# Last 64 keys of two heads in one transposition and in V's 64x64 quadrants, V's banks moved, all engine lists reordered

## What is computed

```python
# q, k, v: (4, 8, 576, 64) float32; x: (2304, 512); w_in: (512, 2048); w_out: (2048, 512)
q_rot, k_rot = (rotate(q), rotate(k))            # rotary embedding
scores = scale * np.matmul(q_rot, k_rot.transpose(0, 1, 3, 2))
scores = scores - np.max(scores, axis=-1, keepdims=True)
attn = np.exp(scores)
attn = attn / (np.sum(attn, axis=-1, keepdims=True) + 1e-09)
x = np.matmul(attn, v)                           # then to (2304, 512)
h = x @ w_in
sp = np.where(h > 20.0, h, np.log1p(np.exp(np.minimum(h, 20.0))))
g = h * np.tanh(sp)
return (g @ w_out).astype(np.float32)
```

## Time and profile before

| | us |
|---|---|
| median of 3 runs | 639.99 (636.27 to 640.86) |
| the profiled execution | 638.16 |
| its span, first to last instruction | 635.3 |
| attention, to the MLP's first matmul | 238.05 |

### The profile page before, as it was taken

How to read it: one execution, slowest core, us unless ns; L and a number is a source line. 1 busy time by engine, 2 the same in 40 slices (tenths; PEclk the granted TensorE clock), 3 DMA queues, 4 the chain that set the end, 5 groups by cost and what they waited for, 6 DMA issues and landing times.

```text
span 635.3 us, 12674 instructions
## 1 busy us (share of the span) xinstructions
PE 613.1 (97%) x4548; PEld 472.6 (74%) x4548; DVE 337.3 (53%) x573; ACT 430.0 (68%) x693; POOL 260.4 (41%) x208
## 2 busy tenths in 40 slices
PE   3899999999999979999999999999999999999997
PEld 1566666666666659978888888888888888888886
DVE  3777777687788655773433534433434335144331
ACT  2778778787778746757857558665488574586663
POOL 4877688676797368994000620001420006000000
PEclk9999999999999999999999999999999999999999
DMA  5676676576676445130000060000420000000001
GB/s 193 196 227 203 213 214 195 175 211 209 214 214 203 112 130 144 47 87 33 1 0 1 0 166 35 0 1 0 120 78 0 0 0 0 33 33 0 0 0 66
DMA packets 39343, 59.61 MB, mean 94 GB/s; under 512 B 4880, under 2 KB 25104, under 8 KB 39312
## 3 DMA queue, kind: packets, MB, share of 16 engines
q1 hardware_dynamic: 39312, 59.20, 31.2%
HBM read 42.60 MB, written 9.51 MB: 82 GB/s over the span
## 4 chain that ended last, share of the span: by engine, by line
PE 68%; POOL 17%; issue 7%; DMA 3%; SPq 2%; ACT 1%; DVE 1%; POOLq 0%; DVEq 0%; ACTq 0%
PE ps_y L754 10%; PE ps_y L756 10%; PE ps_y L755 10%; PE ps_h L732 9%; PE ps_h L730 9%; PE ps_h L731 9%; POOL raw L492 8%; PE ps_s L622 5%; PE ps_s L679 5%; POOL qk_a L500 2%; PE ps_t L649 2%; POOL win_lo L515 2%; DMA xb_l<-r_early 1%; POOL wout_lo L562 1%; POOL xb_l L556 1%
## 5 line engine op out<-in xcount | busy, mean ns | idle before, releaser
L1032 DVE TENSOR_TENSOR h_sb<-h_sb,m_sb 128x1024 f32<-128x1024 f32 x36 | 55.5, 1542 | 145.5 <-ACT m_sb L893 145.5
L960 DVE TENSOR_SCALAR_CACHE_REDUCE minus_s<-ps_s 128x576 f32<-128x576 f32 x144 | 106.1, 753 | 38.7 <-PE ps_s L622 37.5
L820 ACT ACTIVATE prob<-minus_s,neg_max 128x576 f32<-128x576 f32 x128 | 97.9, 768 | 29.1 <-DVE minus_s L960 29.0
L622 PE MATMUL ps_s<-qk_b,qk_a 64*128 64x288 f32 (+1 forms) x320 | 101.0, 445 | 12.7 <-DMA qk_b<-qk_a 11.0
L754 PE MATMUL ps_y<-wout_hi,gh 128*128 128x512 f32 x288 | 112.2, 389 | 0.5 <-POOL wout_lo L562 0.5
L756 PE MATMUL ps_y<-wout_hi,gl 128*128 128x512 f32 x288 | 112.1, 389 | 0.0
L755 PE MATMUL ps_y<-wout_lo,gh 128*128 128x512 f32 x288 | 112.0, 389 | 0.0
L492 POOL TENSOR_TENSOR raw<-raw,rope_t 128x576 f32<-128x576 f32 x62 | 86.8, 1421 | 49.5 <-DMA raw<-qk_in 49.5
L622 PE MATMUL ps_s<-qk_a,qk_b 64*128 64x288 f32 (+1 forms) x320 | 101.1, 445 | 0.0
L730 PE MATMUL ps_h<-xb_h,win_hi 128*128 128x512 f32 x256 | 99.6, 389 | 0.0
L731 PE MATMUL ps_h<-xb_l,win_hi 128*128 128x512 f32 x256 | 99.6, 389 | 0.0
(11 more groups left out here) (65 smaller groups left out, 1023.8 us busy)
## 6 DMA issues: line engine op xcount, KB each, us to landing
raw<-qk_in SPq DMA_DIRECT2D x32, 576.0 KB, 4.1
v_st<-v_in SPq DMA_DIRECT2D x32, 160.0 KB, 2.8
qk_b<-qk_a SPq DMA_DIRECT2D x32, 144.0 KB, 2.5
x_transposed<-xt SPq DMA_DIRECT2D x64, 72.0 KB, 3.1
y_out<-y_sb SPq DMA_DIRECT2D x18, 256.0 KB, 2.0
win_raw<-w_in SPq DMA_DIRECT2D x16, 256.0 KB, 4.9
wout_raw<-w_out SPq DMA_DIRECT2D x16, 256.0 KB, 4.8
x_raw<-x_transposed SPq DMA_DIRECT2D x4, 1024.0 KB, 5.6
```

The costliest lines, as they stand in the source:

```text
L622: return nc.tensor.matmul(out, q[rows, e, m, cols], k[rows, e, m, r * SIDE:(r + 1) * SIDE], start=True, stop=True)
L820: nc.scalar.activation(dst, minus_s[:, ring(word)].rearrange("p a k -> p (a k)"), ACT.Exp, bias=neg_max[:, col:col + 1], scale=-1.0, accum ...
L960: nc.vector.tensor_scalar(minus_s[:, ring(word)], ps_s[:, score_buf(word, m), :, 0:SIDE], -1.0, None, ALU.mult, ALU.min, accum_out=neg_max ...
```

## The change

The input's layout changes so that both heads' last 64 keys can share 128 partitions: head b's keys are rolled by 64, its last 64 keys come first, and lie in `prob` right behind head a's last 64. `prob` holds a's 576 columns and b's side by side. One `G4` of 8 transposes turns both heads' last keys at once: a's land on partitions 0 to 63, b's on 64 to 127, in one slot of `pt`. The rotary table gets an own version for b and so doubles.

`Va` and `Vb` become `V0` to `V3` (key tiles 0 and 1 of a, 2 and 3 of a, the same of b; 8 passes each) and `Vt`: six matmuls in 64x64 quadrants that add both heads' last 64 keys. Both heads' sums stay open from `V0` to `Vt`, in the two banks of turning pair 0, which `G0a` also uses; `G4`, `G0b`, `G1b`, `TQ` and `G1a` use pair 1. The score buffers serve only scores. ACT copies x for both heads (`Xa`, `Xb`). The signals change with it: `pt_read` after each half of V, one `pv_done` for both heads after `Vt`. SP issues all moves and raw loads, then the weights, then both V loads and four stores. The word lists of PE, ACT and DVE are ordered anew; POOL puts the sum of a's rotation behind the split of `w_in` and keeps the sums of the pair before.

```diff
-KEYS = tuple(P * t for t in range(4)) + (S - P,)
-PE_STEP = "S0a S1a G1b- S2a S3a G0b- ST Va- S0b G4b- S1b G1a S2b G0a S3b Vb- G4a TQ".split()
-ACT_STEP = "S0a S1a G0b- G1b- S2a S3a Va- G4b- ST S0b S1b S2b G0a G1a S3b G4a TQ".split()
-DVE_STEP = "S0a S1a S2a S3a G1b- ST G0b- S0b G4b- S1b S2b G1a S3b G0a Vb- G4a TQ".split()
+PE_STEP = "S0a ST V0- V1- G4- S1a G0b- S2a S3a G1b- V2- V3- S0b S1b TQ Vt- S2b S3b G0a G1a".split()
+ACT_STEP = "G4- S0a G0b- ST G1b- S1a S2a S3a Xa- Xb- TQ S0b G0a G1a S1b S2b S3b".split()
+DVE_STEP = "S0a ST G4- S1a G0b- S2a G1b- S3a S0b S1b TQ S2b S3b G0a G1a".split()
+TURN_PAIR = {"V": 0, "G4-": 1, "G0b-": 1, "G1b-": 1, "TQ": 1, "G0a": 0, "G1a": 1}
...
-        rope_t = sb0("rope_t", [P, 2, S])
+        rope_t = sb0("rope_t", [P, 2, 2, S])
...
-        prob = sb1("prob", [P, 2, 4, S])
-        prob_t = sb1("prob_t", [P, S])
+        prob = sb1("prob", [P, 4, 2 * S])
+        prob_t = sb1("prob_t", [P, D + S + D])
...
             def first_half(n, m):
+                for e in range(2):
+                    if real(n + 1):
+                        move_qk(e, n + 1, 1 - m)
+                    if real(n + 2):
+                        load_raw(e, n + 2)
+                if real(n):
+                    load_w(n, m)
...
             def second_half(n, m):
                 if real(n):
+                    for e in range(2):
+                        load_v(e, n)
                 if real(n - 1):
+                    for e in range(2):
+                        store_x(e, n - 1)
...
                 if e == 2:
-                    pe.wait_ge(qk_moved[1], 32 * (p + 1))
+                    for head in range(2):
+                        pe.wait_ge(qk_moved[head], 32 * (p + 1))
...
+            def turn_ends(p, banks):
+                for e in range(2):
+                    pe.wait_ge(exp_done[e], 4 * (p + 1))
+                turns_begin()
+                for t in range(4):
+                    for half in range(2):
+                        rows = slice(half * D, half * D + D)
+                        mm = nc.tensor.transpose(ps_t[:, banks, half, t * D:t * D + D], prob[rows, t, FULL:FULL + P],
+                                                 id_f[rows, rows])
+                mm.then_inc(ends_turned, 1)
...
+            def ends_times_v(p):
+                pe.wait_ge(ends_taken_a, p + 1)
+                pe.wait_ge(ends_taken_v, p + 1)
+                products_begin()
+                for first, count, side, own in ((0, SIDE, 0, False), (SIDE, FULL - SIDE, 1, False), (FULL, D, 1, True)):
+                    for e in range(2):
+                        rows = slice(e * D, e * D + D)
+                        mm = nc.tensor.matmul(x_part(e, side, first - side * SIDE, count), v_st[rows, e, 4, :],
+                                              pt[rows, e if own else 0, 4, first:first + count],
+                                              start=False, stop=(own or side == 0))
+                mm.then_inc(pv_done, 1)
...
-            def take_x(word, p, m):
-                act.wait_ge(pv_done[0], p + 1)
+            def take_x(e, p):
+                act.wait_ge(pv_done, p + 1)
                 if due(p):
+                    act.wait_ge(x_stored[e], 32 * p)
...
+    table[1, :, 1] = np.roll(table[1, :, 1], D, 2)
...
+    both[1::2, 1] = np.roll(both[1::2, 1], D, 2)
```

More of the change, by code:

```diff
@@ L151, in place, with main_key, earlier_score, earlier_turn @@
 def place(step, word):
-    mine = [w for w in step if w[0] == "G" and w[2:] == word[2:]]
+    mine = [w for w in step if w[:2] in ("G0", "G1") and w[2:] == word[2:]]
     return mine.index(word)
-def earlier_user(users, word, n, back):
-    at = users.index(word)
-    while True:
-        at -= back
-        if at < 0:
-            at, n = at + len(users), n - 1
-        if real(n + shift(users[at])):
-            return users[at], n + shift(users[at])
-        if isinstance(n, int) and n < -3:
-            return None
+def main_key(e, kt):
+    return e * (S + D) + kt * P
+def earlier_score(word, n):
+    at = SCORES.index(word) - 2
+    if at < 0:
+        at, n = at + len(SCORES), n - 1
+    return (SCORES[at], n) if real(n) else None
+def earlier_turn(word, n):
+    same = [w for w in TURN_ORDER if TURN_PAIR[w] == TURN_PAIR[word]]
+    at = same.index(word)
+    for _ in same:
+        at -= 1
+        if at < 0:
+            at, n = at + len(same), n - 1
+        p = n + (-1 if same[at] == "V" else shift(same[at]))
+        if real(p):
+            return same[at], p
+    return None
 def attention_mlp(nc, qk_d, v_d, w_in, w_out, rope, ident, out):
@@ L424, in load_r @@
                 if b == 1:
[L425 to L426 removed]
+                    sp.wait_ge(pv_done, PAIRS)
                 elif b > 1:
@@ L678, in p_times_v @@
+            def p_times_v(part, p):
+                e, half = part // 2, part % 2
+                group = next(w for w in PE_STEP if w.rstrip("-") == f"G{half}{'ab'[e]}")
+                wait_taken(group, p)
+                if half == 0:
+                    pe.wait_ge(tails_taken_a if e == 0 else tails_taken_v, p + 1)
+                    pe.wait_ge(v_loaded[e], 16 * (p + 1))
+                for kt in (2 * half, 2 * half + 1):
                     for side in range(2):
-                        mm = nc.tensor.matmul(ps_s[side * D:side * D + D, buf, 0, 0:SIDE], v_st[:, e, kt, :],
+                        mm = nc.tensor.matmul(x_part(e, side, 0, SIDE), v_st[:, e, kt, :],
@@ L1097, in by_key_tile @@
     tiles[:, :, 0:4] = heads[:, 0:FULL].reshape(HEADS, 4, P, D).transpose(0, 2, 1, 3)
-    tiles[:, D:P, 4] = heads[:, FULL:S]
+    for e in range(2):
+        tiles[e::2, e * D:e * D + D, 4] = heads[e::2, FULL:S]
     return tiles
```

269 lines of the change are left out of this document (139 added, 130 removed).

## The result

The change made the kernel slower by two thirds of a per cent. That is inside the 1% that I had called no change, with a chance of 0.25, but on the other side of it than forecast: at 644.15 us the changed kernel is 14 us above the 630 of the prediction and 4 above the top of its range.

A forecast was written before the change was run, and what follows sets the result against it. TensorE was taken to bound the kernel, with gains only in the first 238 us. Steps -12.3, start +3.2 and end -0.2 gave -9.3: 628.9 by the profiled execution, 630.7 against the median, stated as 630, range 620 to 640.

The forecast's parts named there:

- The start: Up to step 1's first word: doubled table, a pause and a later ST move it from 23.36 to 26.6, +3.2 us.
- the pause behind `S0a`: In the start, TensorE stands some 3 us behind S0a, as ST now wants both heads' q and k.
- step 1's `ST` waiting for head b's copy: At the start's end, ST wants head b of pair 1, whose copy lands at about 27.2.
- V0 wants the V loads, issued when `Vt` ends: Each step: load takes 3.06 at the median, hidden with 0.15 to spare; 0.05 per step added for slow landings.
- The steady step: Attention loop: 12.75 us per step, 0.88 less than 13.63; over 14 steps -12.3 us.
- my sum: TensorE's words of the new steady step, priced from starts in the old trace: 12.4 us, 0.65 less than 13.0.
- The rule that I weighed against the change: Changing tiling mode drains TensorE; seven shape changes for five cost 0.1 to 0.3 per step, already in the 12.4.
- my walk: Waits followed through the new step's word order: G4 about 0.05, G0b 0.17, V loads 0.05, G1b and G0a none.
- Just hidden: G0a's wait for the copies of x: 0.95 after Vt's end, covered by S2b and S3b at 1.03.
- V's quadrants: Vt's six matmuls in 64x64 quadrants run four abreast and take 0.60 us; about 0.97 with only two abreast.
- evictions don't keep up: Rival, 13%: four of five turns share bank pair 1; G0b, G1b, G0a wait 0.5 more per step, 637.5 us.
- The end: Step 15's start to the MLP: 23.1 plus 0.6 for V loads behind reciprocal stores, 23.7 us, so -0.2.

The follow-up runs named there:

- e9: The changed kernel with GpSimd clearing the new zero columns beside prob_t at the very start, not behind three rotations: 644.96 us in one run.
- e1: The changed kernel with pair 0's two V loads issued right behind pair 1's raw q and k load: 641.29 us, ratio 1.0037 to the kernel before.
- e10: As e7, with GpSimd starting at pair 1, VectorE rotating both heads of pair 0, zero columns first, identity behind the raw loads: 634.27 us, ratio 0.9933.
- e11: The kernel before with ST and G0b exchanged on TensorE, meant to add one change of tile shape: 642.72 us in one run.
- e7: The changed kernel with three corrections together, those of e1, e4 and e5: 636.57 us, ratio 0.9968 to the kernel before.
- e4: The changed kernel with head b's copy of x moved from ScalarE to VectorE, ahead of TQ: 642.26 us, ratio 1.0060 to the kernel before.
- e5: The changed kernel with SP's end reordered: step 15's V loads before reciprocal stores, MLP's second load before the last x stores: 642.50 us, ratio 1.0046.
- e2: The changed kernel with Vt moved on TensorE from behind TQ to right behind V3: 644.22 us, ratio 1.0080 to the kernel before.
- e8: As e7, with G0b behind S1a and S2a and G1b behind S3a and S0b on TensorE: 637.35 us, ratio 0.9976 to the kernel before.

## Why the prediction was wrong

**The start: size right, reasons partly wrong.** 26.65 where I said 26.6. The table is there with 1.27 (I said 1.5 to 1.6), the pause behind `S0a` with 2.88 (3). But I had step 1's `ST` waiting for head b's copy, and it didn't: `TQ` before it waited for GpSimd's cleared columns, an edit that I had not costed at all. e9 shows that both end at about the same time, so the number came out right by luck. It was luck a second time: e1's trace, where `TQ` starts at the same time (24.22, in after 24.29), has 28.15, by the clock. The landing at 27.2 that I named was right: e10 has `ST` at 27.08 behind that very load.

**Step 1: a place never looked at.** -0.9 predicted, +4.6 measured. My step "V0 wants the V loads, issued when `Vt` ends" holds for the loop. For pair 0 nothing has to be waited for, and there the order of SP's list decides: the change put V's load behind two weights, raw loads and moves, and V's product from mid step to its start. Before, head a's load was issued at 19.81; now both were issued at 26.86 and wanted at 28, and I had put this wait at nothing. It is the largest error that a look at the list would have avoided, and in e1 step 1 took 12.91. About 1.0 of the 4.6 is pace, by which I mean the speed of TensorE's passes: 16 passes in 3.09 and not 2.09 behind the stop. TensorE: Matmul & The Clock Gate (the Trainium skill, Part 1) has a clock of two levels that falls after idling; the trace agrees, with 0.88 in that window and 1.00 in the loop.

**The steady step: mechanism right, three terms too small.** 13.29 for 12.75, so -4.6 for -11.4. Word by word, the waits taken out:

- Words: 12.85 in place of 12.38. `S0a` before `ST` takes 0.68 (0.54 in my sum), `TQ` before `Vt` 0.40 (0.31), `Vt` 0.65 (0.60), two scores behind `Vt` 1.08 (1.03), `G4` 0.30 (0.25), each two V words 2.09 (2.06), `ST` with its way out 0.65 (0.73). `G4` behind a V product costs 0.30 in before as well (131.80 to 132.10); I had taken the 0.24 of one behind a score. I had priced the way out of a shape where before had one, and nothing for the ways into `ST` and `Vt`. The rule that I weighed against the change, from TensorEngine Tiling (Array Packing) (the Trainium skill, Key Properties), that a change of mode drains, was right in direction: I said that the price of two more was already in my sum, and most of it was not. About 0.35 of the 0.47 stands at such borders. That is read from distances between starts; no run took a border away by itself, and e11, which was to add one, could be read at one place only.
- `G0b` behind `G4`: 0.28 in this step, 0.19 in the next (in e7 0.27 and 0.19 in turn), 0.17 in my walk.
- `G0a` behind the copies of x: 0.24. "Just hidden", I said, with 0.95 against 1.03. The two copies ended 0.96 after `Vt`'s end (121.97 to 122.93), but `G0a` came 0.36 later still: the way of the signal, which I had left out at this place. e4 showed it by taking it away.
- Unplaced: the steps still differ by 0.17 in turn. In e7 the longer one has 0.08 more at `G0b` and 0.08 more at `S2a` and `S3a`, which looks like waits; why they come in every second step stays open.

What I said of V's quadrants (0.60, measured 0.65) and of V's load in the loop (no wait in after's trace) held. The rival "evictions don't keep up" was right in kind: `G0a` and `G0b` wait 0.43 to 0.52 in sum, some 0.3 more than in my walk; I had given it 13% and 0.5 more per step.

**The end: +2.0 for -0.2.** I had 0.6 for V loads behind the stores of the reciprocals (measured 0.83), and 0.9 each from `G4` to `G0b` and on to `G1b` (measured 1.02 and 1.55). I had put at nothing the lower clock behind these waits (0.94 in that window) and the MLP's second load, which SP issues behind the last stores of x, so that it waits until x is there. The MLP was +1.2 with no edit in it. e5 returned 1.2 at the end and 2.1 in the MLP. What the lower clock cost isn't separated: from V2 to `Vt` after takes 3.48 and e5, at a clock of 1.00, 3.52, since e5 stands for the reciprocals there.

**Sum.** The ledger's error is 15.8 (+6.5 for -9.3): 0.1 at the start, 5.5 in step 1, 6.8 in steps 2 to 14, 2.2 at the end, 1.2 in the MLP. With the three corrections e7's trace has a span of 631.7, where the prediction's own sum gives 635.3 - 9.3 = 626.0. The 5.7 that remain are 0.44 per step over 13 steps, 0.2 of step 1, 0.6 at the end, less 0.85 that the MLP gained. That trace is of e7's fastest run; by the medians 6.6 remain (636.57 for 630). So two steps of the prediction failed, each with about half of the error: the price of the new step (12.75, measured 13.29, of which 0.17 was the copy that e4 moved), and the loads that SP's list issues late at the first step and at the end, with the lower clock behind the waits, of which I had counted only the 0.6.

## What to carry to other kernels

Where a product or a load is moved, walk the queue that issues it once for the first step and once for the last, not only for the steady one: here three misplaced entries in SP's list cost over 6 us by the traces of e1 and e5 (3.4 by their ratios), where the steady steps gained 4.6. A change of tile shape has a price at each border, into the new shape as much as out of it, so count borders before counting saved passes. When one wait is moved off a copy, look for the engine that is next at its limit: here VectorE's 0.68 per row maximum took over in e2 and e8, where scores were placed closer together.
